# The rounded copy of the gate output is made by VectorE from the first activation, not by a second activation on ScalarE

## The reference

```
y[t]  = r[t] . (state + (u * k[t]) v[t]^T)
state = w * state + k[t] v[t]^T

h1 = x @ w_in1;  x2  = (h1 * 1 / (1 + exp(-1.702 * h1))) @ w_out1
h2 = x2 @ w_in2; out = (h2 * tanh(softplus(h2))) @ w_out2
```

## Time and profile before

| | us |
|---|---|
| median of 3 runs | 915.35 |
| the profiled execution | 916.02 |
| its span, first to last instruction | 914.1 |
| TensorE busy | 883.5 |
| VectorE busy | 333.0 |
| ScalarE busy | 287.7 |
| GpSimd busy | 175.8 |

### The profile page before, as it was taken

How to read it: one execution, slowest core, us unless ns; L and a number is a source line. 1 busy time by engine, 2 the same in 40 slices (tenths; PEclk the granted TensorE clock), 3 DMA queues, 4 the chain that set the end, 5 groups by cost and what they waited for, 6 DMA issues and landing times.

```text
span 914.1 us, 12364 instructions
## 1 busy us (share of the span) xinstructions
PE 883.5 (97%) x4908; PEld 729.9 (80%) x4908; DVE 333.0 (36%) x459; ACT 287.7 (31%) x506; POOL 175.8 (19%) x153
## 2 busy tenths in 40 slices
PE   6489999999999999999999999999999999999998
PEld 5367888888888888888888888888888888888886
DVE  8636724433562464345144422222122122221211
ACT  1333433223222322322254532323322332322322
POOL 4748642522323152222000000000000000000000
PEclk8689999999999999999999999999999999999999
DMA  9764422231242222122422000000000000000000
GB/s 178 165 151 122 91 39 57 49 73 23 52 93 39 45 61 65 31 51 50 143 70 70 1 1 1 34 1 1 35 1 1 34 1 1 35 1 1 34 1 35
DMA packets 54792, 44.26 MB, mean 48 GB/s; under 512 B 30288, under 2 KB 49360, under 8 KB 54736
## 3 DMA queue, kind: packets, MB, share of 16 engines
q1 hardware_dynamic: 52448, 41.90, 19.0%
q10 hardware_dynamic: 2288, 1.57, 0.9%
HBM read 36.37 MB, written 4.72 MB: 45 GB/s over the span
## 4 chain that ended last, share of the span: by engine, by line
PE 89%; SPq 3%; POOL 2%; DMA 2%; DVE 1%; issue 1%; ACT 0%; DVEq 0%
PE h L831 42%; PE acc L850 41%; PE a_bank L752 2%; PE y_bank L771 2%; PE y_bank L783 2%; DMA mid<-in_r 2%; SPq L301 1%; SPq L293 1%; DMA arena<-in_r 1%; PE a_bank L796 1%; POOL arena L401 1%; SPq L271 0%; SPq L266 0%; POOL arena L390 0%; POOL arena L403 0%
## 5 line engine op out<-in xcount | busy, mean ns | idle before, releaser
L668 DVE TENSOR_TENSOR g_lo<-act,g_hi 128x512 fp32r<-128x512 f32 x192 | 174.5, 910 | 511.5 <-ACT g_hi L499 511.5
L831 PE MATMUL h<-xs,win_hi 128*128 128x512 f32 x1152 | 336.0, 395 | 9.6 <-DMA xs<-xs 9.6
L831 PEld LDWEIGHTS h<-xs,win_hi 128*128 128x128 f32 x1152 | 214.1, 189 | 56.3 <-issue 10.5
L496 ACT ACTIVATE act<-h 128x512 f32<-128x512 f32 x192 | 114.8, 598 | 270.1 <-PE h L831 270.0
L499 ACT ACTIVATE g_hi<-h 128x512 fp32r<-128x512 f32 x192 | 114.9, 598 | 256.1 <-PE acc L850 256.1
L850 PE MATMUL acc<-g_hi,wout_hi 128*128 128x512 f32 x576 | 165.7, 389 | 0.0
L850 PE MATMUL acc<-g_hi,wout_lo 128*128 128x512 f32 x576 | 165.6, 389 | 0.0
L850 PE MATMUL acc<-g_lo,wout_hi 128*128 128x512 f32 x576 | 165.6, 389 | 0.0
L831 PE MATMUL h<-xs,win_lo 128*128 128x512 f32 x576 | 163.1, 391 | 0.0
L831 PEld LDWEIGHTS h<-xs,win_lo 128*128 128x128 f32 x576 | 108.5, 188 | 23.4
L850 PEld LDWEIGHTS acc<-g_hi,wout_hi 128*128 128x128 f32 x576 | 108.1, 188 | 22.5
(11 more groups left out here) (94 smaller groups left out, 444.2 us busy)
## 6 DMA issues: line engine op xcount, KB each, us to landing
arena<-in_rk SPq DMA_DIRECT2D x44, 192.0 KB, 3.5
arena<-in_wts SPq DMA_DIRECT2D x16, 384.0 KB, 3.5
arena<-in_k SPq DMA_DIRECT2D x22, 192.0 KB, 4.2
arena<-in_v SPq DMA_DIRECT2D x22, 192.0 KB, 4.0
arena<-in_r SPq DMA_DIRECT2D x21, 192.0 KB, 3.7
out<-mid SPq DMA_DIRECT2D x5, 768.0 KB, 3.3
xs<-xs SPq DMA_DIRECT2D x144, 16.0 KB, 1.8
mid<-in_wts SPq DMA_DIRECT2D x3, 768.0 KB, 5.0
```

The costliest lines, as they stand in the source:

```text
L496: act.activation(act1[:, f % 2], h_bank[f % 2][:, :], GATES[layer])
L668: dve.tensor_tensor(g_lo[:, f % 2], act1[:, f % 2], f32(g_hi[:, f % 2]), ALU.subtract).then_inc(glo_done, 1)
L831: ins = pe.matmul(hb, w[:, f, kd, :], x_part(lo, par, kd), start=i + kd == 0, stop=i == 2 and kd == KD - 1)
```

## The change

The second activation (L499) and its wait for `g_used` go. `g_done` now counts the first activation, the one into `act1`. VectorE, in `split_g`, waits for `g_done` and `g_used` as before, copies `act1` into `g_hi`, counts a new semaphore `ghi_done`, waits for it and then subtracts. `down` waits for `ghi_done` in place of `g_done`; `up` still waits for `g_done`.

```diff
+        ghi_done = sem("ghi_done")
@@ gate (ScalarE)
-                act.activation(act1[:, f % 2], h_bank[f % 2][:, :], GATES[layer])
-                if t * NF + f >= 2:
-                    act.wait_ge(g_used, t * NF + (f - 1))
-                act.activation(g_hi[:, f % 2], h_bank[f % 2][:, :], GATES[layer]).then_inc(g_done, 1)
+                act.activation(act1[:, f % 2], h_bank[f % 2][:, :], GATES[layer]).then_inc(g_done, 1)
@@ split_g (VectorE)
                 dve.wait_ge(g_done, t * NF + f + 1)
                 if t * NF + f >= 2:
                     dve.wait_ge(g_used, t * NF + (f - 1))
+                dve.tensor_copy(g_hi[:, f % 2], act1[:, f % 2]).then_inc(ghi_done, 1)
+                dve.wait_ge(ghi_done, t * NF + f + 1)
                 dve.tensor_tensor(g_lo[:, f % 2], act1[:, f % 2], f32(g_hi[:, f % 2]), ALU.subtract).then_inc(glo_done, 1)
@@ down (TensorE)
-                pe.wait_ge(g_done, t * NF + f + 1)
+                pe.wait_ge(ghi_done, t * NF + f + 1)
```

## The result

| | before | after |
|---|---|---|
| median, us | 914.59 (6 runs) | 917.78 (6 runs) |
| the profiled execution, us | 916.02 | 921.45 |
| its span, us | 914.1 | 919.5 |

The ratio of the times is 1.0052, 95% interval 1.0032 to 1.0074: the change made the kernel slower by half a percent. No change was forecast, at 914.9 us. The medians of the table are only 3.2 us apart, which would be a ratio of 1.0035. But the six of the table are not typical: the fifteen recorded executions of the changed kernel fall in two groups, eight from 917.2 to 919.1 us and seven from 920.8 to 922.5 us, and five of those six are of the lower group. Over all fifteen the median is 919.1 us, 4.5 us above the kernel before. The profiled execution is of the upper group, so its trace shows more of the loss than a typical one has.

A forecast was written before the change was run, and what follows sets the result against it. TensorE's own instructions were taken to bound the kernel behind about 50 us. All terms were 0 but 0.5 us won in the first tile: 915.35 - 0.5 = 914.9 us for the median, range 912 to 919 us.

The forecast's parts named there:

- The copy's own price: On VectorE, each of 192 added copies takes 0.42 us, 81 us more in all; effect on the end 0.
- the last step: Between the two last `down`s, the last subtraction ends at 907.95, ahead of its first reader at 909.08; cost 0.
- the moves of x: The second tile's last moves may be issued 0.5 to 1.3 us later, with 5 us of cover; cost 0.
- Rival 3: TensorE runs faster without ScalarE's 192 reads of PSUM; 906 us if 1% came off, chance 0.03.
- rival 4: The copy isn't the fast one, 0.69 us or more in place of 0.42; even then 915 us, chance 0.03.
- The first tile: Earlier rounding starts GpSimd's run 1.9 us sooner there; 0.5 us won, bounds 1.4 us won to 1.5 us lost.
- Beside GpSimd: At 240 us GpSimd may stop copy and subtraction; the sum into the state keeps 1.1 us of room; effect 0.
- The signs of being wrong: TensorE waiting at `down` for copy or subtraction, or for the sum behind 115 us; or nine matmuls under 2.04 us.
- a sign of being right: In TensorE's list of waits, no new entry, and the three waits in the first tile down to one.
- The first rival: Stopped copy and subtraction make the sum into the state late in 12 batches behind the first tile; 921 us, chance 0.07.
- The second: `g_hi` itself comes late for `down`, if the copy ends 8.4 us after it could start; 919 us, chance 0.03.
- The 0.5 us won: In the first tile, ScalarE rounds weights earlier, so two of TensorE's three waits for the sum go; 0.5 us faster.

The follow-up runs named there:

- old gate in tile 0: The changed kernel, with both activations and no copy for blocks 0 to 16, the change kept for the other 175: 914.58 us, ratio 1.0003.
- the repeat: The changed kernel measured once more, unaltered, against the kernel before: 919.98 us, ratio 1.0059.
- rounding between: The kernel before, with ScalarE's rounding of the weights in the first tile put between the two activations, no copy on VectorE: 913.89 us, ratio 0.9996.
- ScalarE waits: The changed kernel, with ScalarE's old wait for `g_used` put back behind its one activation: 916.19 us, ratio 1.0014.
- gaps on GpSimd: The changed kernel, with GpSimd waiting for copies at two points of each attention batch beside the first tile: 914.28 us, ratio 1.0001.

## Why the prediction was wrong

**The copy's own price** was right (0.42 us reckoned, 0.43 median), ScalarE's 115 us worth nothing was right, and so were the last step, the moves of x and the eleven later tiles, to 0.1 us each. The old gate in tile 0 alone shows that (1.0003). Rival 3 is out, as the tiles behind the first are as long as before, and rival 4, as the copy was the fast one.

**The step that failed** is "The first tile", with the part "Beside GpSimd" that fed it. The mechanism had been found there: GpSimd stops the subtraction, would stop the copy, and the sum into the state is the next thing late. It was then sized at one place only, the batch at 240 us, where GpSimd's run is four operations and 5.3 us and the sum has 2.4 us of room. In the first tile the run was nine operations and 10.0 us, and the room is nil: the scores were late there already, by 0.2 us. The prediction counted the first tile's copies only as what they take from GpSimd, "0.4 us a turn", with a bound of -1.5 us. What they cost was what GpSimd's run takes from them: 8.25 us in one stop, 3.56 and 3.00 in two others. What the prediction had won there was real as far as GpSimd goes: counted from the tile's start, the ageing at 85.27 was done 1.5 us sooner than its twin before (37.3 us against 38.7). But the sum then waited for VectorE and no longer for GpSimd. The profiled execution lost 6.7 us in that tile, and the medians 3.2 and, in the repeat, 5.9 us, against a bound of 1.5.

The range given, 912 to 919 us, holds the first of the two medians (917.78) but not the second (919.98), and it reached so high only for the rivals' sake. The signs of being wrong looked for a late sum behind 115 us alone; the longest wait ended at 109.18, so they would have missed it. What did not come true is a sign of being right: the three waits in the first tile stayed three.

**The first rival** named what happened, at 0.07, but with a condition that was wrong (two stops of a whole run; one sufficed) and in the wrong batches (the twelve behind the first tile, not the second and third in it). The second happened only once, at 0.2 us, where the sum was put first.

**The 0.5 us won** by the earlier rounding show in the one trace of "rounding between" (first tile 79.4 us against 79.9), though not beyond the noise of its times. In the changed kernel they turned over: the earlier start of GpSimd's run is part of what makes the copies meet it. ScalarE waits against after shows the share, 1.0014 against 1.0052.

**Open.** Which boundary between two GpSimd operations lets VectorE in is not settled. The length of GpSimd's run doesn't settle it either. The kernel before has a run of eleven operations at the same place, 12.8 us from 95.42, longer than the nine after the change, and there the subtraction got in behind the L401 at 97.81 and took 1.68 us (VectorE and GpSimd, kernel before):

```profile
99.04 1.68 DVE L668 TENSOR_TENSOR g_lo<-act,g_hi 128x512 fp32r<-128x512 f32 x1 [2.06 <-ACT g_hi L499]
...
97.81 2.37 POOL L401 TENSOR_TENSOR arena<-arena 112x1024 f32<-112x1024 f32 x1
...
100.14 1.46 POOL L390 TENSOR_TENSOR arena<-arena 128x384 f32<-128x384 f32 x1
```

After the change the copy did not get in behind the same operation, though it had stood there for 0.4 us. So the trace of before doesn't foretell a stop of 8.25 us at that place; it does show that a stop there has no room behind it. A wait that GpSimd really has to sit through lets it in (gaps on GpSimd). Nor was it tried what the two groups of executions hang on. Part of the spread lies ahead of the first tile, which began at 47.0 to 49.4 us in the fourteen traces.

## What to carry to other kernels

Before work is moved to an engine that another can stop, take the longest gap-free run of that other engine in the whole trace as the bound of a stop, not a typical one, and ask what waits behind the moved instruction there. A stop costs by what is queued behind it, not by the result of the instruction itself: here the block that the stopped copy wrote was first read at 113.78, 6.7 us after the copy's end, and the sum queued behind it had no room at all. Where VectorE must copy beside a busy GpSimd, a slower instruction that isn't stopped can be the cheaper one: here a reduce of 686 ns in place of a copy of 427.

## What the runs showed of the hardware that was not expected

VectorE was not let in at the end of the GpSimd operation that held it: the copy stood through eight more, 8.25 us in all. That is longer than the rule in the Trainium skill (SBUF — State Buffer, Who interferes with whom) says, which speaks of one instruction; the measurement decides. GpSimd was held less in turn: its L402, 2.4 us as a rule, took 3.43 us at 77.49 in the kernel after, where VectorE's diagonal (L627) had begun before it. And a wait of 3.7 us in the middle of a busy stretch cost TensorE about 1.6 us more behind it, at the lower clock.
